# An attention and two-MoE kernel on one core: the last up batch laid out anew, the up stage's batch loop written out, and the v part of the second MoE pipelined on VectorE

## The reference, cut to what matters

```
# attention (8 batches, 8 heads, 576 rows, head size 64), no softmax
kv = k^T v;  out = q kv;  out = out / rms(out) * g_norm        # -> x [8, 576, 512]
# first MoE
h = x^T @ U @ V                                                 # rank 32, mixes the 576 rows
u = x + h^T
x2 = u + relu(u @ w_ch1) @ w_ch2                                # 512 -> 2048 -> 512
# second MoE
h = gelu_tanh(x2 @ w_in);  u, v = halves of h                   # 512 -> 1024
v_n = layer norm of v, times g_ln
v_s = w_sg @ v_n + b_sg                                         # mixes the 576 rows
out = x2 + (u * v_s) @ w_out
```

## Time and profile before

| what | value |
|---|---|
| three runs | 1322.26, 1322.92, 1325.2 us; median 1322.92 |
| the profiled execution's own time | 1322.69 us |
| its span | 1320.8 us |
| PE, DVE, ACT, POOL busy | 1279.0, 831.5, 566.5, 93.8 us |
| mean granted clock of TensorE | 0.992 |
| instructions in the span | 22274 |

### The profile page before, as it was taken

How to read it: one execution, slowest core, us unless ns; L and a number is a source line. 1 busy time by engine, 2 the same in 40 slices (tenths; PEclk the granted TensorE clock), 3 DMA queues, 4 the chain that set the end, 5 groups by cost and what they waited for, 6 DMA issues and landing times.

```text
span 1320.8 us, 22274 instructions
## 1 busy us (share of the span) xinstructions
PE 1279.0 (97%) x8446; PEld 1236.4 (94%) x8446; DVE 831.5 (63%) x1172; ACT 566.5 (43%) x920; POOL 93.8 (7%) x107
## 2 busy tenths in 40 slices
PE   5899999999999997999999999999999999999998
PEld 5799999999999997999999999998898998998987
DVE  5865454545445456898888888985654645547443
ACT  4665554545555544544445445534222312222220
POOL 6210000000000000000000000001110210111100
PEclk9899999999999998999999999999999999999999
DMA  9545545444555455753817355362243151350321
GB/s 231 141 149 171 156 150 158 145 144 153 156 167 154 135 173 189 269 180 108 266 51 255 118 199 187 131 178 66 48 97 90 26 119 45 70 119 24 91 57 40
DMA packets 253831, 178.66 MB, mean 135 GB/s; under 512 B 165920, under 2 KB 224304, under 8 KB 253760
## 3 DMA queue, kind: packets, MB, share of 16 engines
q1 hardware_dynamic: 250800, 172.81, 43.7%
q0 software_dynamic: 1600, 4.56, 1.3%
q10 hardware_dynamic: 1360, 0.30, 0.1%
HBM read 109.47 MB, written 66.06 MB: 133 GB/s over the span
## 4 chain that ended last, share of the span: by engine, by line
PE 67%; issue 22%; DVE 4%; POOL 3%; ACT 2%; DMA 1%; SPq 1%; POOLq 0%; DVEq 0%; ACTq 0%
PE ps L1394 19%; PE ps L1396 19%; PE ps L1395 19%; PE ps L1415 2%; PE ps L1399 2%; PE ps L1423 2%; POOL rs L666 1%; POOL x_lo L660 1%; PE ps L1431 1%; PE ps L1442 1%; DMA wc_raw<-in_moe_w_out 1%; DMA v_raw<-in_v 0%; DVE w L1035 0%; PE ps L1425 0%; DVE bn L1292 0%
## 5 line engine op out<-in xcount | busy, mean ns | idle before, releaser
L1394 PE MATMUL ps<-x_hi,w 128*128 128x288 f32 x896 | 271.1, 303 | 11.1 <-DVE h_st L1073 7.4
L1395 PE MATMUL ps<-x_lo,w 128*128 128x288 f32 x896 | 265.4, 296 | 0.0
L1396 PE MATMUL ps<-x_hi,w 128*128 128x288 f32 x896 | 265.0, 296 | 0.0
L1394 PE MATMUL ps<-r_hi,w_hi 128*128 128x384 f32 x672 | 224.6, 334 | 0.5 <-DVE r_lo L1189 0.5
L1396 PE MATMUL ps<-r_hi,w_lo 128*128 128x384 f32 x672 | 224.5, 334 | 0.0
L1395 PE MATMUL ps<-r_lo,w_hi 128*128 128x384 f32 x672 | 224.5, 334 | 0.0
L867 ACT ACTIVATE r_hi<-hb 128x768 fp32r<-128x768 f32 x168 | 142.4, 848 | 168.6 <-PE ps L1396 164.0
L1394 PEld LDWEIGHTS ps<-x_hi,w 128*128 128x128 f32 x896 | 169.7, 189 | 12.6 <-DVE h_st L1073 7.9
L1395 PEld LDWEIGHTS ps<-x_lo,w 128*128 128x128 f32 x896 | 169.9, 190 | 0.0
L1396 PEld LDWEIGHTS ps<-x_hi,w 128*128 128x128 f32 x896 | 169.8, 189 | 0.0
L1073 DVE TENSOR_TENSOR h_st<-ps,h_st 128x576 f32<-128x576 f32 x96 | 72.5, 756 | 105.5 <-PE ps L1396 105.4
(11 more groups left out here) (157 smaller groups left out, 2405.5 us busy)
## 6 DMA issues: line engine op xcount, KB each, us to landing
hT_scratch<-h_st SPq DMA_DIRECT2D x64, 576.0 KB, 4.2
hb<-hT_scratch SPq DMA_DIRECT2D x24, 1536.0 KB, 7.4
uT_scratch<-x_raw SPq DMA_DIRECT2D x32, 288.0 KB, 2.3
x_st<-uT_scratch SPq DMA_DIRECT2D x24, 384.0 KB, 3.5
x2T_scratch<-x_st SPq DMA_DIRECT2D x24, 384.0 KB, 6.8
x_raw<-x2T_scratch SPq DMA_DIRECT2D x8, 1152.0 KB, 5.8
xt_in<-x2T_scratch SPq DMA_DIRECT2D x144, 64.0 KB, 2.6
k_raw<-in_k SPq DMA_DIRECT2D x64, 128.0 KB, 2.8
```

Of the source, the lines that this page charges most:

```text
L1394: mm(dst, ws[0], xs[0], start=first, stop=False, skip_group_check=chained)
L1395: mm(dst, ws[0], xs[1], start=False, stop=False, skip_group_check=chained)
L1396: return mm(dst, ws[1], xs[0], start=False, stop=last, skip_group_check=chained)
```

## The change

It has three parts.

1. **Last up batch.** SyncE loads quarters 21 and 22 of `w_ch2` before quarter 11. `w2_sum(0)` no longer waits for quarter 11, `w2_sum(1)` does. The four sums move from steps 11, 13, 15, 17 to 16, 19, 26, 36; the low parts of the weights from 24, 26, 38 to 28, 30, 40; the low parts of h from 44, 45, 46, 48 to 43, 44, 52, 54; the sums of h from 50, 52, 53, 54 to 49, 50, 53, 55. On ScalarE the first two weight high parts move from 20, 22 to 22, 24 and the four pieces of h from 36, 38, 40, 48 to 38, 40, 48, 50.
2. **Up loop.** Batches 1 to 5 are written out on ScalarE, VectorE and TensorE.
3. **v part.** VectorE's order becomes stats(j), normalise(j - 1), low(j - 2); behind the last statistics come normalise(last), then the evacuation of the first out tile of the batch before (not in the first batch), then the last two `low`. The other out tiles are evacuated where all of them were before.

```diff
--- before.py
+++ after.py
@@ -443,9 +443,9 @@
                 sp.wait_ge(s_ust[r], 16 * B)
             up_steps(B - 1, 0)
             store_h(B - 2, NG - 1)
-            load_w2(w2_raw[0], 0, 0, 0)
             load_w2(w2_raw[4], 1, 0, 1)
             load_w2(w2_raw[5], 2, 1, 1)
+            load_w2(w2_raw[0], 0, 0, 0)
             load_w2(w2_raw[6], 3, 1, 0)
             store_h(B - 1, 0)
             up_steps(B - 1, 4 * NI)
@@ -836,10 +836,8 @@
                         x_high(t + 1, 1 - par, X_HIGH_AT.index(k))
 
             up_tile(0, 0, first=True)
-            with act.Fori(0, B // 2 - 2) as i:
-                up_tile(2 * i + 1, 1)
-                up_tile(2 * i + 2, 0)
-            up_tile(B - 3, 1)
+            for t in range(1, B - 2):
+                up_tile(t, t % 2)
             up_tile(B - 2, 0, end=True)
 
             def w2_high(j):
@@ -883,17 +881,17 @@
                         copied(t, k)
                     if k in X_HIGH_THEN:
                         x_high(t, 1, 3 + X_HIGH_THEN.index(k))
-                    if k == 20:
+                    if k == 22:
                         act.wait_ge(s_p, STEPS * t + 2 * NI)
                         w2_high(0)
-                    if k == 22:
+                    if k == 24:
                         w2_high(1)
                     if k == 34:
                         act.wait_ge(s_p, STEPS * t + 4 * NI)
                         w2_high(2)
-                    if k in (36, 38, 40, 48):
-                        h_relu(0, (36, 38, 40, 48).index(k))
-                        h_high(0, (36, 38, 40, 48).index(k))
+                    if k in (38, 40, 48, 50):
+                        h_relu(0, (38, 40, 48, 50).index(k))
+                        h_high(0, (38, 40, 48, 50).index(k))
 
             last_up_tile(B - 1)
             act.wait_ge(s_p, STEPS * B)
@@ -1131,10 +1129,8 @@
                         x_sum(t + 1, 1 - par, {52: 2, 54: 6, 55: 4}[k])
 
             up_tile(0, 0, first=True)
-            with dve.Fori(0, B // 2 - 2) as i:
-                up_tile(2 * i + 1, 1)
-                up_tile(2 * i + 2, 0)
-            up_tile(B - 3, 1)
+            for t in range(1, B - 2):
+                up_tile(t, t % 2)
             up_tile(B - 2, 0, end=True)
 
             W2_ORDER = (0, 1, 2, 4, 5, 3, 6)
@@ -1143,10 +1139,11 @@
 
                 a11, a21, a22, s1, s2, a12 = (w2_raw[j][:] for j in (0, 4, 5, 1, 2, 6))
                 if n == 0:
-                    for i in range(3):
+                    for i in (1, 2):
                         dve.wait_ge(s_w2[i], 16)
                     ins = nc.vector.tensor_tensor(s1, a21, a22, ALU.add)
                 elif n == 1:
+                    dve.wait_ge(s_w2[0], 16)
                     ins = nc.vector.tensor_tensor(a21, a11, a21, ALU.subtract)
                 elif n == 2:
                     dve.wait_ge(s_w2s, 1)
@@ -1198,16 +1195,16 @@
                         added(t, k)
                     if k in X_LOW_THEN:
                         x_low(t, 1, 2 + X_LOW_THEN.index(k))
-                    if k in (11, 13, 15, 17):
-                        w2_sum((11, 13, 15, 17).index(k))
-                    if k in (24, 26, 38):
-                        w2_low((24, 26, 38).index(k))
-                    if k in (44, 45, 46, 48):
-                        if k == 44:
+                    if k in (16, 19, 26, 36):
+                        w2_sum((16, 19, 26, 36).index(k))
+                    if k in (28, 30, 40):
+                        w2_low((28, 30, 40).index(k))
+                    if k in (43, 44, 52, 54):
+                        if k == 43:
                             dve.wait_ge(s_p, STEPS * t + 6 * NI)
-                        h_low(0, (44, 45, 46, 48).index(k))
-                    if k in (50, 52, 53, 54):
-                        h_sum(0, 1, (50, 52, 53, 54).index(k))
+                        h_low(0, (43, 44, 52, 54).index(k))
+                    if k in (49, 50, 53, 55):
+                        h_sum(0, 1, (49, 50, 53, 55).index(k))
 
             last_up_tile(B - 1)
 
@@ -1305,13 +1302,18 @@
                     dve.wait_ge(s_vnhi, NCP * p + j + 1)
                     nc.vector.tensor_tensor(vn_lo[:, j % NJ, :], v_act[:, j % 3, :], vn_hi[:, j % NJ, :].bitcast(F32),
                                             ALU.subtract).then_inc(s_vnlo, 1)
-                for j in range(VB[par], VB[par + 1]):
+                end = VB[par + 1]
+                for j in range(VB[par], end):
                     stats(j)
-                    normalise(j)
                     if j > VB[par]:
-                        low(j - 1)
-                low(VB[par + 1] - 1)
-
+                        normalise(j - 1)
+                    if j > VB[par] + 1:
+                        low(j - 2)
+                normalise(end - 1)
+                if not first:
+                    evacuate(*before(p, par), 0)
+                low(end - 2)
+                low(end - 1)
 
             def us_tile(n):
                 return ps[:, 4 + 2 * (n % 2):6 + 2 * (n % 2), 0:SH]
@@ -1346,12 +1348,15 @@
                         dve.wait_ge(s_ost[i], 16 * slot_uses(i, p, par))
                     nc.vector.transpose(o_st[i][:], xt_in[i % NXT][:]).then_inc(s_xtt, 1)
 
-            def evacuate(p, par):
-                for i in range(batch_tiles(par)):
-                    j = OB[par] + i
-                    dve.wait_ge(s_omm, NCP * p + j + 1)
-                    dve.wait_ge(s_xtt, NCP * p + j + 1)
-                    nc.vector.tensor_tensor(o_st[i][:], ps[:, 2 + j % 2], o_st[i][:], ALU.add).then_inc(s_oev, 1)
+            def evacuate(p, par, i):
+                j = OB[par] + i
+                dve.wait_ge(s_omm, NCP * p + j + 1)
+                dve.wait_ge(s_xtt, NCP * p + j + 1)
+                nc.vector.tensor_tensor(o_st[i][:], ps[:, 2 + j % 2], o_st[i][:], ALU.add).then_inc(s_oev, 1)
+
+            def evacuate_others(p, par, start=1):
+                for i in range(start, batch_tiles(par)):
+                    evacuate(p, par, i)
 
             v_part(0, 0, first=True)
             dve.wait_ge(s_wsl, 80)
@@ -1370,19 +1375,19 @@
             gate(0, 0, first=True)
             with dve.Fori(0, B // 2 - 1) as i:
                 v_part(i, 1)
-                evacuate(i, 0)
+                evacuate_others(i, 0)
                 x2_transposed(i, 1)
                 gate(2 * i + 1, 1)
                 v_part(i + 1, 0)
-                evacuate(i, 1)
+                evacuate_others(i, 1)
                 x2_transposed(i + 1, 0)
                 dve.wait_ge(s_ost[JM], 32 * (i + 1))
                 gate(2 * i + 2, 0)
             v_part(B // 2 - 1, 1)
-            evacuate(B // 2 - 1, 0)
+            evacuate_others(B // 2 - 1, 0)
             x2_transposed(B // 2 - 1, 1)
             gate(B - 1, 1)
-            evacuate(B // 2 - 1, 1)
+            evacuate_others(B // 2 - 1, 1, start=0)
 
 
         @block.tensor
@@ -1533,10 +1538,8 @@
                         attention_step(k, t, first, end)
 
             up_tile(0, 0, first=True)
-            with pe.Fori(0, B // 2 - 2) as i:
-                up_tile(2 * i + 1, 1)
-                up_tile(2 * i + 2, 0)
-            up_tile(B - 3, 1)
+            for t in range(1, B - 2):
+                up_tile(t, t % 2)
             up_tile(B - 2, 0, end=True)
             up_tile(B - 1, 1, final=True)
```

## The result

The changed kernel takes 1307.82 us (median of 4 runs, 1305.61 to 1309.7), the kernel before on the same chip 1323.49 (4 runs, 1322.26 to 1325.2): a ratio of 0.988 with a 95% interval of 0.986 to 0.990. The forecast was 1306.4 in a range of 1304.5 to 1311.5. The profiled execution took 1308.49 us, its span is 1306.7 instead of 1320.8: 14.1 us less, where 16.3 were forecast.

The account below looks back on a forecast made before the run. TensorE was taken as the bound, busy 1279.0 of 1320.8 us, so only its pauses could be won. 9.4 + 2.3 + 4.0 + 0.6 = 16.3 us off 1322.69 gave 1306.4 us, range 1304.5 to 1311.5.

Parts of the forecast that it names:

- The last up batch: TensorE's stalls and low clock there cost 10.0 us; 0.6 kept, gain 9.4, bounds 6.4 and 10.0.
- The tightest point: Last up batch, before step 26: additions queued behind the sum awaiting the third load finish with 0.2 us to spare.
- the walk: Step-by-step timing of the last up batch with measured durations, counting what stalls stay: 0.6 us.
- The new stall before step 40: Last up batch: the addition of step 37 waits behind the sum at step 36; 0.5 us, clock kept at 2.4 GHz.
- lands 7.0 us later: Last up batch: the second block of h, asked for after step 41 at 515.7, lands at 522.8.
- Cost 0.1: Last up batch: sums of h push the addition of step 51 to 525.35, wanted by TensorE at 525.3.
- The up loop: Before batch 3: TensorE's taken loop branch loses 2.3 us, won by writing the loop out; bounds 0 and 2.4.
- The v part: Second MoE: seven out-product pauses end, 4.0 us (bounds 3.0 and 4.0); the first batch's w_sg transposes pause goes, 0.6.
- The ring of 3.05 us a tile: v part: GELU, statistics and low wait on each other; rival: out-product stalls stay, 1310.4 us, chance 0.08.
- The late third load: Rival, last up batch: TensorE waits again before step 26, 1 to 3 us; 1308 to 1311.5 us, chance 0.13.
- Written-out code: Rival, up loop: it costs what the branch did, or the pause was not the branch's; 1308.7 us, chance 0.05.
- The instruction stream: Rival, batches 1 to 5: waiting for 20 fresh packets costs 46 us, 1352; decides from 19.1 (16.3 and 2.6); chance 0.02.

Follow-up runs that it names:

- run 6: The changed kernel with the three loads of w_ch2 back in their old order (quarter 11 first), step numbers as changed; 1310.99 us.
- run 9: The changed kernel itself measured once more, nothing edited; 1306.35 us, ratio 0.9869.
- run 10: The changed kernel with sums and low parts of the last up batch moved to steps that leave the additions free; 1306.51 us, ratio 0.9865.
- run 12: run 10 plus a one-column GELU on ScalarE behind the last ReLU, loading GELU's table early; 1303.33 us, ratio 0.9859.
- run 5: The kernel before with only the last up batch's new load order and step numbers; 1315.94 us.
- run 7: The changed kernel with 112 semaphore increments added on TensorE's queue, to shift the instruction packets; 1308.75 us.
- run 8: The changed kernel with 256 semaphore increments added on TensorE's queue, a whole instruction packet; 1306.53 us.
- run 11: run 10 with VectorE's old order in the v part, the evacuation still put forward; 1306.72 us, ratio 0.9867.
- run 1: The kernel before with only TensorE's up loop written out; 1319.19 us.
- run 2: The kernel before with only ScalarE's and VectorE's up loops written out, TensorE's loop kept; 1324.59 us.
- run 3: The kernel before with only the evacuation of the first out tile put forward, VectorE's v part otherwise in its old order; 1317.95 us.
- run 4: The kernel before with only the new order of statistics, normalise and low, all evacuations behind the last low part; 1325.73 us.

## Why the prediction was right

**The last up batch (9.4 forecast, 7.45 in the profile).** The cause was right: additions queued behind sums that waited for a load. Run 6 shows the load's part. The tightest point was where the walk put it, before step 26 (0.2 us of spare forecast; a pause of 0.22 to 0.25 in the profile after and in runs 9, 10 and 12, none in runs 5, 7, 8 and 11). A wait before step 26 was one of the prediction's signs of being wrong; in this size it is the missing spare and no more. The new stall before step 40 was 0.68 us and 0.1 at its restart for the 0.5 forecast, with the clock kept. What failed is a term: "lands 7.0 us later", with the "Cost 0.1" behind it. In the profiled execution the block took 8.1 us and the pause was 1.34; in run 9 it was 7.1 and 0.33. The walk had no spare for it and took one landing for all. Of the 1.95 us that are missing 1.0 is this late landing; the rest is that each of the three pauses takes 0.3 more than forecast (0.23 and 0.1 for none, 0.68 and 0.1 for 0.5, and 0.33 and 0.1 for 0.1 as in run 9), so the walk was short by 0.3 at each of its three tight points.

**The up loop (2.3 forecast, 2.39 between starts).** The landmark of step 19 shows 1.37 only, because this execution's prologue was 1.03 us longer: the first matmul of the up stage behind a wait starts at 68.49, where it started at 67.46, and the diff touches nothing before it. This landmark wanders from execution to execution: 66.83, 67.00, 67.40, 65.96 and 68.92 in runs 1 to 5, which change nothing in front of it either, and 67.15 in run 9 of the changed kernel. Runs 1 and 2 show TensorE's loop as the cause, against the name in the profile. The sum without this term, 14.0, lies beside the 14.2 us of this one execution, but that is chance: the pause of 2.3 us is gone in run 1, where only TensorE's loop was changed. The Trainium skill (Advanced Engine Details and Errata, Control Flow Timing) gives about 108 ns for a compare-and-branch; the one taken here took 3.99 us in run 2.

**The v part (4.0 and 0.6 forecast; 4.9 in the second MoE).** The seven pauses went, 4.2 us in run 3, and it was the evacuation put forward that ended them, not the pipeline; run 4 shows the pipeline alone making them longer. The small pause at the transposes of w_sg is gone as well, and that is the pipeline's part, worth 0.6. The ring of 3.05 us a tile was 2.99 (989.60 less 986.61 for the statistics), the fifth GELU 0.85 us late for 1.0. The prediction feared that the root and the low part beside it would hold each other up. They did not. GpSimd's root, all executions of the line (ns of shortest, median, longest), first in the kernel before and then in the changed one:
```profile
L666 POOL TENSOR_TENSOR rs<-ve,half_neg x36: 549/550/569, 894.9 to 1264.8; 128x1 f32<-128x1 f32 x36
```
```profile
L666 POOL TENSOR_TENSOR rs<-ve,half_neg x36: 548/782/791, 885.7 to 1251.1; 128x1 f32<-128x1 f32 x36
```
The root stretched, from 0.55 to 0.78 us, and VectorE's low part kept its 0.68. But it is not the low part that stretches it: in the changed kernel each root starts 0.16 us behind the start of a normalise, except the first of each batch. The eight roots that have only a normalise beside them take 0.78 to 0.79 us, the twenty that also meet a low part 0.78, and the first ones, with neither, 0.55 to 0.57. VectorE reads the root only one tile later, so it costs nothing.

**Sum.** The profiled execution: 1.4 + 7.45 + 5.3 = 14.1, for 16.3 forecast. Its missing 2.2 us are 1.0 of the prologue and 1.0 of one landing; the 0.9 by which the three pauses were set too small is nearly made good by 0.8 more than forecast in the up loop and behind the last up batch. That these two cancel is luck. Neither the long prologue nor the late landing was there in the repeat (67.15 for the landmark, 0.33 us of pause), whose profiled span lay 16.4 below that of the profile before. The two pairs of medians differ by 15.7 and 17.1 us. They were not taken apart run by run; falls of the clock behind short pauses (below) can be in them, and neither the sum nor the bounds had these.

**The rivals.** The late third load did not come, though 0.2 us of pause says how close it was. The ring did not keep the stalls. Written-out code did not cost what the branch did (run 1). The instruction stream was not slow, and it was not new either. The pages count its packets, first before and then after:
```profile
q8 instruction: 49, 0.80, 0.2%
```
```profile
q8 instruction: 47, 0.77, 0.2%
```
The loop of before fetched its instructions again on its second pass, 22 packets from 119 to 425 us where the written-out code takes 20. So the "20 packets of fresh instructions" were no addition, and this rival had nothing to stand on. (Its bound of 19.1 us is 18.9 by the two terms that it names.)

## What to carry to other kernels

Where an engine waits for a short operation, read what its queue holds ahead of it: here three additions stood behind sums that waited for a load, and an evacuation behind two low parts that nobody needed for 20 us. Moving the one operation that releases the bound engine was worth 4.2 us; pipelining the chain around it, done alone, made the pauses longer. Walk the steps with measured durations, and give a transfer that has no spare the spread of its landings rather than one of them; and look at where a function table is loaded, since 1.28 us in front of an awaited operation can be moved into idle time with one column.

## What the runs showed of the hardware that was not expected

- **The length of a short pause does not decide whether the clock falls.** TensorE fell to 1.2 GHz for some 3.4 us behind pauses of 1.92 us (run 10), 2.01 (run 11), 2.25 (run 2, before batch 3), 2.38 (run 7) and 2.5 (run 4, before the third v tile, and run 6), but not behind 2.25 at the same place before batch 3 in run 4, 2.27 (kernel before, runs 3 and 5), 2.18 (run 6, at 887 us) or 1.83 (runs 2 and 9). Each fall costs about 1.7 us (in run 10 the starts of 512 columns are 0.43 us apart instead of 0.23), more than most single edits here.
- **The prologue** wanders by 3.0 us (65.96 in run 4 to 68.92 in run 5 for the landmark of the first batch), in code that no edit touched. With the clock this is the other part of the scatter that was found, and 1.0 us of run 12's profile (66.52) against run 10's (67.51) is of this kind. Its cause is open.
- **The taken branch** took 4.0 us on TensorE's queue where it jumps back over two up batches, and 0.22 in the down loop, whose body is shorter. In the kernel before the first kind was followed by packets of instructions on the whole second pass (the first 1.7 us behind the branch's start), while the down loop, from its second pass to the last, took no packet (none from 648 to 904 us). This fits a body that has to be fetched again against one that does not; the size of the body was not varied, so it is not shown.
- **GpSimd's root** stretched from 0.55 to 0.78 us behind a normalise of 128x512 that had started 0.16 us before it, and the normalise kept its 0.54. Beside GpSimd's x_lo it is VectorE that stretches: all seven long executions of line 1336 (0.76 to between 2.25 and 5.47 us) have an x_lo under way that started before them.
- **A load of 1.5 MB** (a block of h) landed in 6.8 to 7.2 us in 39 of 42 cases and in 8.0, 8.1 and 9.0 in three, those with a packet of instructions fetched 4.9 to 5.8 us behind the issue (run 9).
